# Attention with 16-bit values that carry gate columns, routing for pairs of tiles, and regrouped weight work

## The reference

```python
def _attn_ref(q, kv, w_sr):                       # q: 2 x 12288 x 128, kv: 2 x 384 x 32 x 128
    kv_pool = kv.reshape(B, H // r, r, W // r, r, C).mean(axis=(2, 4))      # r = 4
    k = v = kv_pool.reshape(B, -1, C) @ w_sr                                # 768 keys
    s = (q @ k.transpose(0, 2, 1)) / sqrt(C)
    a = exp(s - s.max(-1));  a /= a.sum(-1) + 1e-09
    return a @ v

def _moe_ref(x, w_gate, w1, w2):                  # 8 experts, 128 -> 1024 -> 128
    logits = x @ w_gate;  e = argmax(logits);  gate_w = softmax(logits)[e]
    return gate_w * (maximum(x @ w1[e], 0) @ w2[e])

# then _moe2_ref: the same with logits = normalised x @ normalised expert_emb.T / tau
```

## Time and profile before

| | |
|---|---|
| median of 3 runs | 2017.84 us (2016.92 to 2021.18) |
| the profiled execution's own time | 2017.97 us |
| its span in the trace | 2016.2 us |
| keys and values, until | 93 us |
| attention, until | 795 us |
| first expert stage, until | about 1436 us |
| last expert stage, until | 2016 us |
| PE busy | 1881.2 us, 93% |

### The profile page before, as it was taken

The page is one execution under the profiler, slowest core; times in us unless marked ns, Lnnn a source line. Parts: engine busy times, 40 slices in busy tenths (PEclk is TensorE's granted clock), DMA queues, the critical chain, the costliest instruction groups (busy, mean ns, idle before and its releaser), DMA issues. The chain is left out here.

```text
span 2016.2 us, 62408 instructions
## 1 busy us (share of the span) xinstructions
PE 1881.2 (93%) x16614; PEld 1641.2 (81%) x16615; DVE 1477.3 (73%) x4042; ACT 1239.1 (61%) x3079; POOL 738.5 (37%) x1100
## 2 busy tenths in 40 slices
PE   4799999999999995999999999999499999999998
PEld 3678878878787884888888888888499999989997
DVE  6578999968888874677877777776466666666666
ACT  1266666657777773677777766666355555555555
POOL 0003333333333334154444454545433333333333
PEclk9699999989999996999999999999699999999999
DMA  9402433312333312133333311111111111111110
GB/s 224 127 21 81 122 112 109 102 40 66 100 120 105 118 41 71 28 92 101 97 107 107 98 45 46 45 44 30 47 50 51 47 47 47 43 47 49 49 47 27
DMA packets 131599, 148.78 MB, mean 74 GB/s; under 512 B 33070, under 2 KB 102842, under 8 KB 131520
## 3 DMA queue, kind: packets, MB, share of 16 engines
q1 hardware_dynamic: 90944, 87.57, 16.0%
q0 software_dynamic: 19328, 38.19, 5.7%
q10 hardware_dynamic: 21248, 22.04, 3.5%
HBM read 90.41 MB, written 42.39 MB: 66 GB/s over the span
## 5 line engine op out<-in xcount | busy, mean ns | idle before, releaser
L1862 DVE SCALAR_TENSOR_TENSOR hT_l<-ps_hidden,hT_l 128x512 f16<-128x512 f32 x412 | 283.1, 689 | 184.9 <-ACT hT_l L1819 161.5
L1568 DVE SCALAR_TENSOR_TENSOR hT_l<-ps_hidden,hT_l 128x512 f16<-128x512 f32 x412 | 282.6, 686 | 135.8 <-ACT hT_l L1514 124.6
L1819 ACT ACTIVATE hT_l<-ps_hidden 128x512 f16<-128x512 f32 x412 | 240.0, 597 | 229.8 <-PE ps_hidden L1761 228.5
L1514 ACT ACTIVATE hT_l<-ps_hidden 128x512 f16<-128x512 f32 x412 | 245.4, 596 | 179.0 <-PE ps_hidden L1447 123.1
L1901 POOL DMA_INDIRECT out<-out_rows_l,out_slots_l x206 | 200.5, 973 | 381.0 <-DVE out_rows_l L1870 342.2
L1761 PE MATMUL ps_hidden<-xT_l,W 128*128 128x256 f16 x2472 | 339.0, 274 | 1.0 <-DVE xT_l L1848 1.0
L1447 PE MATMUL ps_hidden<-xT_l,W 128*128 128x256 f16 x2472 | 338.4, 273 | 1.1 <-DVE xT_l L1563 1.1
L624 POOL DMA_INDIRECT rows<-att_rows,att_slots x192 | 188.1, 980 | 395.1 <-ACT exps L969 344.1
L1461 PE MATMUL ps_y<-W,hT_l 128*128 x1648 | 307.1, 279 | 8.7 <-DVE hT_l L1568 8.6
L1775 PE MATMUL ps_y<-W,hT_l 128*128 x1648 | 293.8, 273 | 1.2 <-DVE hT_l L1862 1.2
L907 PE MATMUL ps_out<-expsT,V 128*128 128x512 f32 x864 | 274.4, 426 | 0.3 <-ACT oT L979 0.3
(11 more groups left out here) (190 smaller groups left out, 3113.0 us busy)
## 6 DMA issues: line engine op xcount, KB each, us to landing
x_l<-rows SPq DMA_DIRECT2D x206, 130.0 KB, 2.1
w_chunk<-in_moe_w SPq DMA_DIRECT2D x48, 512.0 KB
kv_raw<-in_kv SPq DMA_DIRECT2D x16, 768.0 KB, 10.0
q<-in_q SPq DMA_DIRECT2D x48, 256.0 KB
W<-weight_parts SPq DMA_DIRECT2D x16, 512.0 KB, 3.5
w_chunk<-in_moe_w ACTq DMA_DIRECT2D x16, 512.0 KB
W<-weight_parts ACTq DMA_DIRECT2D x16, 512.0 KB, 3.0
w_raw<-in_moe_w ACTq DMA_DIRECT2D x8, 512.0 KB, 10.3
```

Of the source, the lines that this page charges most:

```text
L1514: nc.scalar.activation(hT[:, p, 0, :], psH[:, (HP * h + p) % HB, :], ACT.Relu).then_inc(h_high, 1)
L1568: nc.vector.scalar_tensor_tensor(out=hT[:, p, 1, :], in0=psH[:, (HP * h + p) % HB, :], scalar=0.0, in1=hT[:, p, 0, :], op0=ALU.max, op1=AL ...
L1819: nc.scalar.activation(hT[:, p, 0, :], psH[:, p, :], ACT.Relu).then_inc(h_high, 1)
L1862: nc.vector.scalar_tensor_tensor(out=hT[:, p, 1, :], in0=psH[:, p, :], scalar=0.0, in1=hT[:, p, 0, :], op0=ALU.max, op1=ALU.subtract).then ...
```

## The change

- **Values.** `keys_and_values` multiplies `w_sr` with the gate weights first (one transpose, one small matmul), and makes for each key 128 value columns and 8 gate columns, kept in fp32 in the space of `W0`. The new class `ValueScales` makes, during the bodies t = 0 and 1, their largest values (DVE), a reduction over the partitions (POOL), scales, and fp16 high parts (ACT, six operations) and low parts (DVE, four). A row of `V` holds 128 values, 8 gate columns, the key's largest value and a one (138 columns), then 136 columns of low parts.
- **Mixing.** The exponentials are fp16 parts and stationary; V streams. Each step has 12 matmuls of 138, 136 and 138 columns in place of 3 of 512; the output is tokens by columns, and brings the gate logits, a bound for the row's size and the denominator along. Mixing of tile t is done whole in body t+2. The matmuls with the gate weights, the transposes of the output, DVE's row maximum, and ACT's running sum of the exponentials are gone. ACT copies the output in two pieces of 276 columns.
- **Routing** (`PairRouter`) is done for two tiles at once (128x64 in place of 128x32), with single buffers: the even body of a pair has the choosing steps, five of them (best to hot) one behind the other in step kb = 3; the odd body the rest. The transposes of q and of the exponentials share two PSUM banks.
- **Weight work.** Sizes are taken one chunk per body, for the first layer in the first loop and for the second in the second; each layer has a reduction of its own (t = 23 and t = 45). In the second loop POOL scales a chunk and makes its low part, ACT makes the high part from the scaled chunk. Loads run one chunk ahead. The pipeline has two more bodies, and the last pass of each loop is written out.

```diff
@@ allocate @@
+    k.v_scale = sb("v_scale", [P, B])
+    k.gate_ratio = sb("gate_ratio", [P, B])
 ...
+    floats = k.W[0][:].bitcast(F32)
+    k.values = floats[:, 0:B * KB * (C + E)].rearrange("p (b x c) -> p b x c", b=B, c=C + E)
@@ class WeightSplit @@
-    def vec_low(self, dve, e, w):
-        dve.wait_ge(self.high, e * 2 + (w + 1))
-        self.nc.vector.scalar_tensor_tensor(
 ...
+    def pool_scale(self, pool, e, w):
+        pool.wait_ge(self.loaded[w], e * 16 + 16)
+        scale = self.k.wscale[:, self.layer, w:w + 1].to_broadcast([P, FF])
+        self.nc.gpsimd.tensor_tensor(self.raw(w), self.raw(w), scale, ALU.mult).then_inc(self.scaled, 1)
+    def act_high_scaled(self, act, e, w):
+        act.wait_ge(self.scaled, e * 2 + (w + 1))
 ...
+        self.nc.scalar.activation(self.parts[:, :, 0, :], self.raw(w).rearrange("p (b c) -> p b c", c=P),
+                                  ACT.Copy).then_inc(self.high, 1)
+    def pool_low(self, pool, e, w):
+        pool.wait_ge(self.high, e * 2 + (w + 1))
+        self.nc.gpsimd.tensor_tensor(self.parts[:, :, 1, :], self.raw(w).rearrange("p (b c) -> p b c", c=P),
+                                     self.parts[:, :, 0, :], ALU.subtract).then_inc(self.low, 1)
@@ keys_and_values @@
+            nc.tensor.transpose(psW[:, 0:C], w_sr[:, 0:C], k.ident[:]).then_inc(w_turned, 1)
+            pe.wait_ge(w_copied, 1)
+            nc.tensor.matmul(psV[:, 0, 0:E], w_srT[:], k.w_gate[:], start=True, stop=True).then_inc(w_turned, 1)
 ...
+                    nc.scalar.activation(k.values[:, b, 3 * h:3 * h + 3, :],
+                                         psV[:, h, 0:3 * (C + E)].rearrange("p (x c) -> p x c", c=C + E),
+                                         ACT.Copy).then_inc(vcopied, 1)
@@ class PairRouter (was Router) @@
+        self.choose = Steps(sem("choose"), ["denominator", "unit", "logits", "best", "gaps", "ranked", "winner", "hot"])
+        self.size = Steps(sem("size"), ["row_floor", "power", "scale"])
 ...
+        if name == "denominator":
+            dve.wait_ge(self.copied, u * 4 + 4)
+            ins = nc.vector.tensor_scalar(self.denom[:], self.Y[:, :, VOUT - 1], 1e-9, k.v_scale[:, b:b + 1], ALU.add,
+                                          ALU.mult)
 ...
+            ins = nc.vector.scalar_tensor_tensor(out=self.lg[:], in0=self.Y[:, :, C:C + E],
+                                                 scalar=k.gate_ratio[:, b:b + 1], in1=repeat(self.unit[:], E),
+                                                 op0=ALU.mult, op1=ALU.mult)
@@ attention @@
-        XT = sb("expsT", [P, 3, 2, TQ], F32R)
-        oT = sb("oT", [P, 2, TQ])
 ...
+        XT = sb("expsT", [P, 2, KB, 2, TQ], F16)
 ...
+        psX = ctx.enter_context(nc.psum_tensor("ps_turn", [P, 2, 512], F32))
+        psO = ctx.enter_context(nc.psum_tensor("ps_out", [P, 2, 512], F32))
+        ranks = psO[:, 0, 2 * VOUT:2 * VOUT + (2 * QS + 1) * E]
@@ attention, sync @@
-                    (sizes, split)[b].sync(sp, e, par)
+                    sizes[b].wait_sized(sp, e, par)
+                    if not isinstance(e, int) or e + 1 < E:
+                        sizes[b].load(sp, e + 1, par)
+                if e is not None and b == 1:
+                    if par == 0:
+                        split.load(sp, e, 1)
+                    elif not isinstance(e, int) or e + 1 < E:
+                        split.load(sp, e + 1, 0)
+                    split.place(sp, e, par)
@@ attention, tensor @@
-            def mix(t, b, kb):
+            def mix(t, par, g, b, kb):
+                pair, part = divmod(kb, KB // 2)
                 if kb == 0:
-                    wait(pe, o_copied, t)
-                pe.wait_ge(x_low, t * KB + (kb + 1))
-                for j, (vp, xp) in enumerate(((0, 0), (0, 1), (1, 0))):
-                    mm = nc.tensor.matmul(psO[:], k.V[:, b, vp, kb, :], XT[:, kb % 3, xp, :],
-                                          start=(kb == 0 and j == 0), stop=(kb == KB - 1 and j == 2))
-                mm.then_inc(mixed, 1)
 ...
-            def body(t, par, b, e):
+                    wait(pe, router.copied, t * 2 - 1)
+                    if par == 1 and routes(g - 2):
+                        router.slotting.wait(pe, g - 2, "advance")
 ...
+                elif part == 0:
+                    wait(pe, router.copied, t * 2)
+                if pair == 0:
+                    pe.wait_ge(x_low, t * KB + (2 * part + 2))
+                for x in (2 * part, 2 * part + 1):
+                    for i in range(2):
+                        s = slice((2 * pair + i) * P, (2 * pair + i + 1) * P)
+                        for xp, v0, n in ((0, 0, VOUT), (0, VOUT, C + E), (1, 0, VOUT)):
+                            mm = nc.tensor.matmul(psO[:, pair, i * VOUT:i * VOUT + n], XT[:, par, x, xp, s],
+                                                  k.V[:, b, x, v0:v0 + n],
+                                                  start=(x == 0 and i == 0 and xp == 0 and v0 == 0),
+                                                  stop=(x == KB - 1 and xp == 1), skip_group_check=True)
+                if part == KB // 2 - 1:
+                    mm.then_inc(mixed, 1)
+            def body(t, par, g, b, e):
                 for kb in range(KB):
                     if has(t, 0):
-                        scores(t, par, t // QT_B if b is None else b, kb)
+                        scores(t, par, batch(t, b), kb)
+                    if has(t, 2):
+                        mix(t - 2, par, g, batch(t - 2, b), kb)
+                    if kb == KB - 1 and par == 0 and routes(g - 2):
+                        pe.wait_ge(router.copied, min(t * 2 - 3, QT * 2) if isinstance(t, int) else t * 2 - 3)
+                        router.pe_rank(pe, g - 2)
                     if has(t, 1):
                         turn_exps(t - 1, 1 - par, kb)
-                    back = 2 if kb < 2 else 1
-                    if has(t, back):
-                        mix(t - back, (t - back) // QT_B if b is None else b, (kb - 2) % KB)
-                    if kb == 0 and has(t, 3):
-                        turn_out(t - 3, 1 - par)
-                    if kb == 3 and has(t, -1):
+                    if kb == 0 and has(t, -1):
                         turn_q(t + 1, 1 - par)
 ...
@@ attention, scalar @@
+            def copy(t, pair, place, before):
+                act.wait_ge(mixed, t * 2 + (pair + 1))
 ...
+                nc.scalar.activation(router.Y[:, at:at + 2, :],
+                                     psO[:, pair, 0:2 * VOUT].rearrange("p (i c) -> p i c", c=VOUT),
+                                     ACT.Copy).then_inc(router.copied, 1)
+            def body(t, par, g, b, e):
                 for kb in range(KB):
+                    if kb == 0 and has(t, 3):
+                        copy(t - 3, 1, 1 - par, g - 3 + par)
+                    if kb == 3 and has(t, 2):
+                        copy(t - 2, 0, par, g - 2)
                     if has(t, 1):
-                        high_x(t - 1, kb)
-                    if kb == 1 and has(t, 2):
-                        act.wait_ge(mixed, t * KB - KB)
-                        wait(act, router.tok_done, t - 3)
-                        nc.scalar.activation(oT[:, par], psO[:], ACT.Copy).then_inc(o_copied, 1)
-                    if kb == 2 and has(t, 3):
-                        router.act_rows(act, t - 3, 1 - par)
+                        high_x(t - 1, 1 - par, kb)
+                    if kb == 0 and has(t, -1):
+                        high_q(t + 1, 1 - par)
                     if has(t, 0):
                         for s in range(QS):
                             if done_at[s] == kb:
                                 exps(t, par, s)
-                    if kb == 3 and has(t, -1):
-                        high_q(t + 1, 1 - par)
-                    if kb == 3 and b == 1:
-                        split.act_high(act, e, par)
-                    if kb == 2 and has(t, 3):
-                        router.act_exps(act, t - 3)
+                    if kb in (1, 2, 4, 5) and routes(g - 2):
+                        router.act_row(act, g - 2, par * QS + (1, 2, 4, 5).index(kb))
+                    if kb == 4 and par == 0 and routes(g - 2):
+                        router.act_exps(act, g - 2)
+                    if kb == 3 and b == 1 and e is not None:
+                        split.act_high_scaled(act, e, par)
@@ attention, vector @@
-                small(t, par, ("logits", 3), ("ranks", 4), ("advance", 4))
-                big(0, [], [("best", 3), ("own", 4), ("row_max", 3)])
-                big(1, [("gaps", 3), ("slot", 4), ("row_floor", 3)],
-                    [("ranked", 3), ("power", 3), ("slot_int", 4), ("winner", 3), ("scale", 3)])
-                big(2, [("hot", 3)], [])
-                if b == 0:
-                    sizes.vec_size(dve, e, par, 0)
-                big(3, [("inverse", 2)], [("exp_sum", 3), ("denominator", 1)])
-                if has(t, -1):
```

(49 more changed lines are left out.)

540 lines of the change are left out of this document (304 added, 236 removed).

## The result

The changed kernel takes 2059.28 us (median; 2049.45 to 2060.11), against 2018.24 us for the kernel before in the same runs. The ratio is 1.019, with a 95% interval of 1.0162 to 1.0218: **slower by 1.9%**, where 1983 us was forecast; whether the loss reaches 2% the interval leaves open. The profiled execution took 2049.45 us, with a span of 2047.6 us; it is the shortest of the four, so what is read from it is a lower bound of the loss. Against the span of 2016.2 us of before, 31.4 us have to be found.

The account below looks back on a forecast made before the run. PE, nearly full in attention, was taken to bound the kernel. Attention 619 against 658 us (-39), end -2, clock +3, DVE steps held by POOL +3 make -35: 2018 - 35 = 1983 us, range 1950 to 2009.

Parts of the forecast that it names:

- PE's floor: PE's own work for one attention tile after the change: 11.7 us, against 13.14 for a plain tile before.
- Rivals 4 and 5: Mixing's stationary loads half hidden (2017 us, no change, chance 0.04), or costing their whole duration (2053 us, chance 0.05).
- The hold at t = 24: Between the loops, DVE's `inverse` waits for POOL's reduction, 7.91 us; predicted to go, -8 us.
- What the floor meets: Chain from a tile's first scores to its third maximum and exponential: even loop body 13.7 us, odd 12.6.
- Rival 2: Chains cost more: idle in each body half a microsecond longer, 23 us more, 2006 us; chance 0.16.
- Loop tiles: Attention tiles in the two loops with weight work: 13.3 us each, 32 of them, 425.6 us.
- rival 3: POOL's large operation keeps a DVE step waiting 1.7 us in 16 bodies: 2007 us, chance 0.08; 3 us already forecast.
- Clock: Longer PE idle in even bodies may bring more spells at 1.2 GHz: +3 us.
- Plain tiles: Attention tiles outside the two loops: 12.2 us each, 13.75 of them, 167.8 us.
- Start: Making the values' scales ahead of the first mixing: between 0 and 6 us, taken as +2.5.
- End: Last scores to next stage: 35.5 us against 37.7, so -2, with 16 scatters from about 12.5 us on.
- rival 1: PE sets the pace after all: shorter chain, loop tiles 12.2 us, 35 us less, 1948 us; chance 0.17.

Follow-up runs that it names:

- e1: Changed kernel with the five choosing steps moved on DVE from step kb = 3 to the end of kb = 2: ratio 1.0003 to the kernel before.
- e10: Changed kernel with 8 filler matmuls on PE ahead of step kb = 5's mixing in even bodies: ratio 1.0134 to the kernel before.
- e11: e7 with ACT's high part of a weight chunk moved from step kb = 3 to the end of kb = 4: ratio 0.9885 to the kernel before.
- e3: Changed kernel with the choosing steps and the weight chunk's maximum both moved on DVE out of step kb = 3: ratio 0.9835 to the kernel before.
- e6: e3 with the first block's maximum moved on DVE right behind step 0's low part: ratio 0.9795 to the kernel before.
- e7: e6 with the first block's exponential moved on ACT ahead of step 1's high part: ratio 0.9809 to the kernel before.

## Why the prediction was wrong

**What it had right.** PE's floor, nearly: mixing 0.73 us for twelve matmuls (0.72 predicted), a step 1.88 (1.87), a tile 11.9 (11.7). With it falls the rule of the Trainium skill ("TensorE: Matmul & The Clock Gate", "Back-to-back issue gap") that was weighed against the trace: 81 ns would have made 0.97. Rivals 4 and 5 are out. The hold at t = 24 is gone: the six tiles between the loops take 77.7 us, not 87.7. And the mechanism: the third maximum behind five dependent steps and a weight chunk, which PE waits for through the exponential.

**The step that failed is the laid-out chain ("What the floor meets").** Its sizes, against the even body at 321.81:

| from the body's first scores | predicted | measured |
|---|---|---|
| step 3's transposes end | 8.1 | 8.8 |
| ACT's high part ends | 8.7 | 9.5 |
| DVE's low part ends | 9.4 | 10.2 |
| five steps end | 10.5 | 11.5 |
| third maximum starts | 11.8 | 13.0 |
| its exponential ends: the body | 13.7 | 14.9 |

The large operations last what was laid out (high part 0.60, low part 0.69, maximum and exponential together 1.9); the 1.2 us that are missing lie between them, where the prediction put next to nothing. 0.7 us are lost before the row even starts: the chain took PE's first three steps to run without a wait, but the scores of step 3 wait for the first exponential (0.18 us idle at 328.50, 0.45 by starts), step 0 takes 0.2 longer, with its transposes just behind the fourth exponential, and 0.1 is passage. The five steps take 1.3 from the low part's end, not 1.1, as `hot` starts 0.19 us late; and the short pauses around the weight chunk cost 0.2. Odd bodies miss by nearly the same amount, 13.7 for 12.6. Rival 2 had this mechanism, "chains cost more", at 0.5 us a body and 0.16 chance; without the clock's part it is 1.0 us in each of 32 loop bodies. The reason that it gave, single routing buffers, is not borne out: e1 takes the choosing steps earlier and shortens the bodies all the same.

The deeper slip was in the frame. Before, a loop tile took 13.83 us with about the same operations on DVE. That this was because they stood between large ones and PE had work to give is argued from the orders, and no run shows it. The prediction counted 1.8 us of wait in even bodies, saw PE's floor fall by 1.4 us, and still called the sum a gain, since only the laid-out minimum of the chain was put against a measured mean. A chain that is laid out by hand should have been laid out for before as well, and its error, against 13.83, carried over.

**Terms of the sum, in us (predicted, measured by the profiles):**
- Loop tiles: 13.3 each; 14.3 in the first loop without low clock (e10), so 32 x 1.0 = 32 too low.
- Second loop: 3 for POOL and DVE; it takes 13 us more than the first in e10 (241.9 against 228.9). The lock of rival 3 is a part of it (below); ACT's 1.05 us for a weight chunk's high part is another (e11 shows that it can't be put just anywhere).
- Clock: +3; some 11 by e10.
- Plain tiles: 12.2; 12.6 for tiles 2 to 5 and 12.95 for the six between the loops, 6 in all.
- Start: +2.5; +7.2 with tiles 0 and 1. The time to the first maximum alone varies from 102.0 to 109.1 us over the profiles of the experiments, none of which touches it, so a part of this is chance.
- End: -2; +8.3. The estimate had 16 scatters start 12.5 us behind the last scores. Timeline of POOL in the changed kernel:

```profile
799.71 0.20 POOL L630 TENSOR_TENSOR att_rows<-att_fpart,att_gate 128x4 f32<-128x4 f32 x1 [7.51 <-DVE att_gate L704]
800.82 1.01 POOL L646 DMA_INDIRECT rows<-att_rows,att_slots  x1 [0.91 <-DVE att_slots L720]
...
823.29 0.97 POOL L646 DMA_INDIRECT rows<-att_rows,att_slots  x1 [0.31 <-issue]
826.15 0.10 POOL L1804 MEMSET grp_half<- 128x6 f32 x1 [1.89 <-POOLq L880]
```

POOL stands idle 7.51 us for the gate of the last pair but one, begins the last 16 scatters 19.4 us behind the last maximum (781.4), and needs 22.5 us from the first to the last, since fills stand between them.

With 3 of the second loop and of the clock already in the forecast, these come to 71 us, where 66 were missed (-35 forecast, +31.4 measured); they were taken from different runs.

The range ended at 2009 us; a chance of 0.87 for a gain was much too high for a sum whose largest term was a chain without a single measured counterpart.

**What the change is worth.** e3 is 0.9835 and e6 0.9795 with the same mixing, the same routing for pairs and the same weight work on POOL. So the loss came from where two pieces of DVE work were put. That e3 meets the forecast's ratio (1983 of 2018, 0.983) is chance: the forecast had the wait in it. For a kernel without the wait the prediction's own figure is rival 1's 1948 us, 0.965, and the best version here gains little more than half of that. What keeps the rest, in e7's profile: 12.5 us a tile in the first loop and 13.2 in the second, not 12.2, the later first maxima, and the end of the stage.

## What to carry to other kernels

When PE's work shrinks, what stands ahead of a double buffer's release decides: find the operation that frees the buffer (here the third maximum and its exponential), and keep dependent small steps and riders such as weight maxima out of the row ahead of it, in a place where the engine is idle anyway. A chain laid out by hand came out 1.2 us too short here: lay the old kernel's out too, compare it with its measured period, and carry that error into the forecast. And allow for more than the wait itself where PE waits two microseconds or more: here a stretch at half clock followed in nine cases of fifteen.
